# The last 64 of 320 features in a three-term split product: a 64-row contraction becomes a 128-row one

## Time and profile before

| what | us |
|---|---|
| median of 3 executions | 399.35 (395.54 to 402.44) |
| span of the profiled execution, first to last instruction | 410.3 |
| TensorE matmul busy | 364.5 (89%) |
| TensorE weight load busy | 313.0 (76%) |
| VectorE busy | 257.5 (63%) |
| ScalarE busy | 168.9 (41%) |
| GpSimd busy | 126.2 (31%) |

### The profile page before, as it was taken

The page is one execution under the profiler, slowest core; times in us unless marked ns, Lnnn a source line. Parts: engine busy times, 40 slices in busy tenths (PEclk is TensorE's granted clock), DMA queues, the critical chain, the costliest instruction groups (busy, mean ns, idle before and its releaser), DMA issues.

```text
span 410.3 us, 5465 instructions
## 1 busy us (share of the span) xinstructions
PE 364.5 (89%) x1882; PEld 313.0 (76%) x1882; DVE 257.5 (63%) x457; ACT 168.9 (41%) x302; POOL 126.2 (31%) x137
## 2 busy tenths in 40 slices
PE   0543779998899798998899999999999999999997
PEld 0433658787787687786579999997787997897897
DVE  5557588998956868857252645898848644664211
ACT  1663846335434443232442123544857324514300
POOL 7224154566626645532620201111402001102100
PEclk9999995569658958588569999999999999999999
DMA  5696232234541352106200021013000000010011
GB/s 148 162 313 204 48 112 85 76 108 132 144 125 46 106 165 88 45 2 194 74 0 0 2 100 55 1 49 96 32 2 0 18 32 2 0 49 1 0 50 48
DMA packets 11662, 29.87 MB, mean 73 GB/s; under 512 B 2213, under 2 KB 6661, under 8 KB 10197
## 3 DMA queue, kind: packets, MB, share of 16 engines
q1 hardware_dynamic: 11636, 29.54, 23.9%
HBM read 26.40 MB, written 1.97 MB: 69 GB/s over the span
## 4 chain that ended last, share of the span: by engine, by line
PE 73%; DVE 9%; DMA 8%; issue 4%; SPq 2%; ACT 1%; POOL 1%; DVEq 0%; ACTq 0%; POOLq 0%
PE ps_v L1092 17%; PE ps_s L1092 12%; PE ps_e L1092 7%; PE ps_in L1092 6%; PE ps_out L1092 6%; PE ps_t L1092 6%; PE ps_z L1092 6%; DMA stk_raw<-in_qk 5%; PE ps_in L1156 5%; DMA mrow<-nml 3%; PE ps_out L1166 2%; PE ps_s L1147 2%; PE ps_z L1175 2%; PE ps_e L1137 1%; DVE xg L885 1%
## 5 line engine op out<-in xcount | busy, mean ns | idle before, releaser
L540 POOL TENSOR_TENSOR kkl<-kr,kkh 128x384 fp32r<-128x384 f32 x16 | 16.7, 1042 | 86.2 <-ACT kkh L700 86.2
L1156 PEld LDWEIGHTS ps_in<-tok,pt 128*128 128x128 f32 x192 | 33.2, 261 | 4.0 <-issue 3.3
L1156 PE MATMUL ps_in<-tok,pt 128*128 128x42 f32 x192 | 36.0, 353 | 0.0
L1137 PE MATMUL ps_e<-mrow,est 104*128 104x512 f32 x24 | 15.8, 660 | 20.4 <-DMA mrow<-nml 17.6
L470 POOL TENSOR_SCALAR_AFFINE_SELECT et<-et 128x512 f32<-128x512 f32 x24 | 16.9, 705 | 51.9 <-ACT et L578 51.9
L1064 DVE TENSOR_TENSOR kr<-kr 128x384 f32<-128x384 f32 x32 | 19.6, 616 | 20.4 <-ACT kr L743 20.3
L1092 PE MATMUL ps_v<-win,xth 128*128 128x512 f32 x60 | 29.9, 573 | 1.2 <-DVE xtl L907 1.2
L570 ACT ACTIVATE stk_hi<-stk_raw,lo_row 120x1024 fp32r<-120x1024 f32 x24 | 27.3, 1141 | 7.5 <-DMA stk_raw<-in_qk 7.5
L1147 PEld LDWEIGHTS ps_s<-stk 120*128 120x128 f32 x96 | 21.3, 283 | 11.1 <-DVE stk L826 7.5
L464 POOL TENSOR_TENSOR stk<-stk_raw,stk_hi 120x1024 fp32r<-120x1024 f32 x11 | 27.1, 2467 | 7.6 <-ACT stk_hi L570 7.6
L814 DVE TENSOR_TENSOR pt<-ps_s,et 128x512 f32<-128x512 f32 x24 | 16.3, 680 | 19.0 <-issue 13.6
(11 more groups left out here) (282 smaller groups left out, 1017.1 us busy)
## 6 DMA issues: line engine op xcount, KB each, us to landing
stk_raw<-in_qk SPq DMA_DIRECT2D x36, 320.0 KB
tok<-in_vk SPq DMA_DIRECT2D x12, 328.0 KB, 3.0
sp_raw<-in_w_sp SPq DMA_DIRECT2D x6, 384.0 KB, 4.3
osig<-in_og SPq DMA_DIRECT2D x2, 960.0 KB, 9.5
out_y<-ob SPq DMA_DIRECT2D x12, 160.0 KB, 1.8
wv_raw<-in_w_v SPq DMA_DIRECT2D x2, 640.0 KB, 4.8
win_raw<-in_w_in SPq DMA_DIRECT2D x2, 512.0 KB, 6.6
wk_raw<-in_w_k SPq DMA_DIRECT2D x2, 512.0 KB, 4.5
```

The costliest lines, as they stand in the source:

```text
L540: gp.tensor_tensor(kkl[a % 2][:, b, :], kr[n % 4][:, :], bits(kkh[a % 2][:, b, :]), ALU.subtract).then_inc(sems["kk_lo_pool"], 1)
L1137: te.matmul(ps_e[:, :], est[:, c, :], mrow[:, b, j, :, :].rearrange("p h t -> p (h t)"), start=True, stop=True).then_inc(sems["expo_mm"], 1)
L1156: last = te.matmul(p_in[:, HH * j + h, :], pt[:, j, h, :], vt[u % 2][:, HH * j + h, :], start=True, stop=True)
```

## The change

The 64-row slices go: the eighth matmul of each of the 72 chains reads all 128 rows of the weight slot and of the low data. It thus adds `w_lo x_lo` for the last 64 features, which was left out before. The number of matmuls, their columns, their order, and all waits are as they were. No other engine's program is touched.

```diff
             def split_rows(w, cols):
                 def tile(part, t):
-                    if t == TL:
-                        return w[:, 4, cols] if part == 0 else w[0:64, 4, cols]
-                    return w[:, t + 2 * part, cols]
+                    return w[:, 4 if t == TL else t + 2 * part, cols]
                 return tile
...
             def x_tiles(g, cols):
                 def tile(part, t):
-                    x = (xth, xtl)[part]
-                    rows = slice(0, 64) if (t == TL and part == 1) else slice(0, 128)
-                    return x[rows, g % 2, t, cols]
+                    return (xth, xtl)[part][:, g % 2, t, cols]
                 return tile
...
                     last = chain(ps[:, 0:NB], parts(
                         split_rows(wk, slice(b * 128, b * 128 + 128)),
-                        lambda part, t: x[0:64, 1, t, :] if (part, t) == (1, TL) else x[:, part, t, :]))
+                        lambda part, t: x[:, part, t, :]))
...
                     pairs = parts(split_rows(wr, slice(0, DM)),
-                                  lambda part, t: x[0:64, 1, t, t_] if (part, t) == (1, TL) else x[:, part, t, t_])
+                                  lambda part, t: x[:, part, t, t_])
```

## The result

The changed kernel took 384.02 us, the median of four executions (381.34 to 385.96), against 400.89 us for before (four, 395.54 to 416.81): 16.9 us less, ratio 0.963 with a 95% interval of 0.954 to 0.972. With these and the executions that ran beside the experiments, before ran 66 times with a median of 402.3 us (quartiles 398.5 and 408.7), and the changed kernel 16 times with 383.5 us (381.4 and 385.0): 18.9 us less, and a much narrower spread. The difference isn't the same all along: at the tenth percentile it is 12.4 us (393.7 and 381.3), at the ninetieth 27.9 (413.7 and 385.7). The ratios leave out executions over 1.5% above the fastest of their kernel, which trims before more than the changed kernel and gave 1.021 (1.007 to 1.035) for before timed against itself, so I judge single microseconds by medians of all executions.

What follows compares the result with a forecast made beforehand. TensorE was taken to bound the second part, sharing the path with a DMA round trip in the first. Savings of 16.9 + 1.7 - 2.2 + 5 = 21.4 us from 399.35 gave 378 us, range 370 to 386.

Steps and rivals of the forecast that it cites:

- What the 64-row matmul costs: In each chain of eight, changing to the 64-row shape and back costs 0.39 us in k, 0.40 in r.
- Rival C: In all chains, the gap isn't due to the shape, so nothing changes: 399 us; chance 0.04.
- k and r, with the gap before k(1): Second part: 44 chains give 16.9 us, less a new 2.2 us TensorE wait for DVE's last shifted tile.
- u(3): Four chains directly ahead of sp(0), one at half clock (0.5 us), three at full (0.4 each): 1.7 us.
- The cover that ends: At k(1)'s start, TensorE comes 4.2 us earlier against 2.0 us of slack, so it stands still for 2.2 us.
- v and u in the slots: First part: of 24 chains, about twelve to fifteen give 0.4 us each; 5 us taken, 2 to 9 as ends.
- The floor of 8.45 us: In the first part's slots, the distance where the `mrow` DMA ends the wait; such slots get no shorter than 8.4 us.
- The base: The profiled execution of before, 410.3 us, 11 us above the median; its saving was subtracted from 399.35 us.
- A: The gap before k(1) lets the clock fall, costing 5 to 10 us: 383 us, up to 388; chance 0.19.
- B: First part: half-clock stretches become shorter, four slots fall about 2 us each, 8 us more: 370 us; chance 0.15.
- D, slower: Shorter slots turn into `mrow` waits and the lower clock holds through the second part: slower by over 2%; chance 0.02.

Runs made afterwards that it cites:

- paired: The kernel before, with odd-numbered k chains beginning with their 64-row matmul, so two stand side by side: 396.86 us against 404.57, ratio 0.989.
- extra_4: The changed kernel with the first matmul of each of the 24 v and u chains in the slots issued five times: 382.16 us against 401.44 for before.
- vu_only: The kernel before with 128 rows only in the 28 v and u chains, k and r keeping the 64-row matmul: 397.16 us, ratio 0.992.

## Why the prediction was right or wrong

- *What the 64-row matmul costs*: right, and the reason too (0.39 us forecast). 0.40 us of a chain of eight (1.79 to 1.39) and 0.40 of an r chain. paired shows that it is the change of shape. Rival C, that it is something else, is out.
- *k and r, with the gap before k(1)*: 16.9 - 2.2 = 14.7 us forecast, 14.9 measured between the cut and the last matmul. The gap was 2.34 us where 2.2 were forecast, on the tile and the engine named, at DVE's pace.
- *u(3)*: 1.7 us forecast, 1.25 measured at the full clock at best (7.17 to 5.92) and 0.14 (7.17 to 7.03) in six of ten profiles, after among them. "The cover that ends" was worked out for the shifted tiles of k(1) and not for `sp_lo` ahead of sp(0), where DVE ends late as well and TensorE waits 1.1 us. The forecast had no such term.
- *v and u in the slots*: this step failed. "There remain about twelve to fifteen chains at 0.4" took the chain of waits of one execution as the list of what TensorE's time is worth, chain by chain at an unchanged clock. extra_4 put 96 matmuls there and nothing got longer, with the clock higher by 0.09. The first part as a whole, 6.7 us with u(3) in the forecast, gave 2.0 in the first four executions (16.9 - 14.9), 4.5 in vu_only, and 4.0 over all executions (18.9 - 14.9). In executions without a long stretch at the half level next to nothing came of it (cuts at 200.0 to 202.8 us with 64 rows, a median of 200.9 without), and what the medians have beyond the second part comes from the long end of before's times: the difference is 12.4 us at the tenth percentile and 27.9 at the ninetieth. So it doesn't come as a sum over chains. That the removed pauses are what keeps the clock up at the end of the first part would fit, and stays open. The floor of 8.45 us for a slot that ends in the DMA wait was a little too high as well: between the exponents at 146.46 and 154.42 us after has 7.96.
- *The base*: the profile of before was an execution whose first part was 13.7 us longer than in another profile of the same code, with 19.5 us at 0.50. Prices per chain at the half clock and the list of slots that TensorE sets were read from stretches that the second profile of the same code doesn't have (0.96 from 110 to 140 us, where this one had 0.73). I had noted that it lay 11 us above the median, and still used its first part for a term.
- *Rivals A and B*: A's mechanism exists, at 1.3 us instead of 5 to 10. B pointed at the half-clock stretches, and they did become rarer in the profiles, without proof that the change is the cause; its 8 us were far too many for a median. D, slower, had no sign in any run.

The range has a slip in its working: with one bound at a time the sums run from 374 to 381 us (the largest step down is 4, the largest up 3), not from 371 to 382.

The forecast of 378 us was 6 us under the 384.0 of the first four executions; 4.7 of these are the first part (6.7 forecast, 2.0 measured), and before's median moved up by 1.5 meanwhile, so by ratio it is 0.947 against 0.963. Over all executions the change is 18.9 us where 21.4 were forecast.

## What to carry to other kernels

Look at the shape column of the weight loads before counting rows or multiply-adds: a slice of 64 rows between fuller ones costs a pause on both sides, here about 0.4 us to a visit, while 96 rows cost none; where the operand's other rows hold something harmless, contract them too, or put the small ones side by side. Where the clock swings, don't price a step from one profiled execution: take a second profile of the same code, and cut the time at a point behind which nearly all executions agree. A chain of waits that names TensorE isn't a proof that its time counts; adding superfluous matmuls there is a cheap test of it, if the granted clock is read beside it, which rose here with the added work (0.82 to 0.91). And when TensorE gets faster, look at each place where it starts to read something new, and ask which engine it used to arrive behind: one such wait was forecast here, the other wasn't.

## What the runs showed of the hardware that wasn't expected

- A 96-row slice takes part in the full shape (337 ns a matmul), a 64-row one doesn't (442 ns).
- Two 64-row matmuls in a row need only one way in and one way out (0.25 us of idle time each in the loads), across two PSUM banks and two accumulations.
- 19 us of additional dense TensorE work in the slots cost no time (cut at 200.28 against 200.51 us), with a mean clock of 0.91 instead of 0.82 from 80 to 200 us.
- A DVE subtraction of 128 x 384 took 1.37 us beside a GpSimd subtraction, 0.55 alone. Where both start at almost the same time it can go either way: two DVE subtractions of 128 x 768 took 2.94 us and GpSimd's of 128 x 512 1.29 (after), or 1.82 and 2.13 (vu_only).
- After an idle time of 2.0 to 2.4 us between dense matmuls the clock fell in two of eleven profiles, and was back early in the second chain of eight.
